# Attention and two gated layers on one Trainium2 core: the setup ahead of the first head, rearranged between VectorE, GpSimd and ScalarE

## The chip, the cores and the metric

The kernel runs on one core of a Trainium2 chip. The metric is the device time of one execution in microseconds (us). A core has TensorE (PE, with its weight loads PEld), VectorE (DVE), ScalarE (ACT), GpSimd (POOL) and SyncE (SP), which here issues the DMAs. The engines run their own instruction lists and wait for one another by semaphores.

## What is computed

Causal attention with a decay bias over 32 heads (4 batches of 8, 576 tokens, head size 64), then two gated layers over 2304 tokens. The part that matters here is the bias, which comes from a running sum over each head's `s`:

```python
scores = scale * np.matmul(q, k.transpose(0, 1, 3, 2))
s_pos = np.maximum(s, 0.0)
cum = np.cumsum(s_pos, axis=-1)
bias = -(cum[:, :, :, None] - cum[:, :, None, :])
scores = np.where(causal, -1000000000.0, scores + np.minimum(bias, 0.0))
scores = scores - np.max(scores, axis=-1, keepdims=True)
attn = np.exp(scores)
attn = attn / (np.sum(attn, axis=-1, keepdims=True) + 1e-09)
x = np.matmul(attn, v)               # then heads side by side: [2304, 512]
h = x @ w_in                         # softmax gate, normalisation, @ w_out
h = maximum(x @ w1, x @ w2, x @ w3)  # second layer, @ w_out2
```

## The kernel before

Every product is made from a high and a low part, so each q, k, v, probability and weight is split in two. One head's attention is spread over three slots of a software pipeline (`slot(t, ...)` on each engine): scores and exponentials of head t, transposes of head t-1, values of head t-2. After the attention come the first layer in six groups of 384 tokens and the second layer in six groups.

The bias is folded into the scores matmul. Four rows beside the 64 rows of q and k in the tile `qk_b` (q_b and k_b are its left and right parts) hold ones, the running sum and its negative, each in high and low parts. For all 32 heads these rows are built once, in the tile `setup` (32 partitions, 8 rows of 576): ones in rows 0, 2, 5, 7 (`one_rows`), `cum_hi` and `cum_lo` in rows 1 and 3, and their negatives `ncum_hi` and `ncum_lo` in rows 4 and 6. The first two heads get their four rows straight from `setup` (L309); the whole tile is then stored to DRAM (L310), and later heads are loaded from there (L299).

Line numbers here are those of the kernel before. Its setup, engine by engine:

- DVE sets the four rows of ones (L1027), waits for `s`, takes its positive part (L1032), makes the running sum with a scan (L1034), splits it (L1036 writes `cum_hi`, L1038 `cum_lo`), then zeroes the 64 columns ahead of `q_a` and `q_b` in both buffers (L1040, L1041). Next is `q_low(0, 0)` (L1047), which waits for POOL's `q_hi_ready`.
- ACT writes `ncum_hi` once `cum_hi` is there (L828) and `ncum_lo` once `cum_lo` is there (L830); each raises `cum_ready`. Its next work is the first exponential (L846).
- POOL zeroes `qk_b` in both buffers (L696, semaphore `rows_zeroed`), zeroes and fills the identities and the mask (L698 to L705), two constants (L707, L708), and then begins on head 0: `qk_high` (L716 q_a, L717 k_a, L718 q_b) and `k_low` (L722), then the same for head 1.
- SP issues `s`, then q/k and v of heads 0 and 1, waits for `rows_zeroed` and for `cum_ready` at 2, and issues the rows of heads 0 and 1 (L309), the store of `setup` (L310) and `g_ln` (L311). `reload(2, ...)` comes after that and waits for POOL's and DVE's splits of head 0.
- PE waits for `setup_pool` at 5 and `setup_dve` at 1. Its first work, `scores_4(0)`, then waits for the high and low parts of q and k of head 0 and for `aux_loaded[0]`, the semaphore of L309.

Of the kernel before, what the change touches and what calls it, by code (L numbers as in the profile page):

```python
# [8 lines left out]
ALU = mybir.AluOpType  # L9
ACT = mybir.ActivationFunctionType  # L10
# [25 lines left out]

def attention_and_mlp(nc, qkT, v, s, w_in, w_out, g_ln, w1, w2, w3, w_out2, out):
    HEADS, D, _, S = qkT.shape
    DM, FF = w_in.shape
    FF2 = w1.shape[1]  # L40
# [4 lines left out]
    PAD = P - S % P  # L45
    NCH = (S + PAD) // P
    SP = S + PAD
# [35 lines left out]
    with ExitStack() as ctx:  # L83
        def sem(name):
            return ctx.enter_context(nc.semaphore(name))
# [7 lines left out]
        def sb(stack, name, shape, dt=F32):  # L93
            return stack.enter_context(nc.sbuf_tensor(name, shape, dt))
# [22 lines left out]
        with ExitStack() as a:  # L117
# [9 lines left out]
            q_a = [sb(a, f"q_a{i}", [P, SP], F32R) for i in range(2)]  # L127
            qk_b = [sb(a, f"qk_b{i}", [P, SP + S], F32R) for i in range(2)]
# [7 lines left out]
        q_b, k_b = [t[:, 0:SP] for t in qk_b], [t[:, SP:SP + S] for t in qk_b]  # L136

        one_rows = [setup[:, i, :] for i in (0, 2, 5, 7)]
        cum_hi, cum_lo, ncum_hi, ncum_lo = [setup[:, i, :] for i in (1, 3, 4, 6)]
# [40 lines left out]
        pool_passed = sem("pool_passed")  # L180
        setup_pool = sem("setup_pool")
        rows_zeroed = sem("rows_zeroed")
        setup_dve = sem("setup_dve")
        cum_step = sem("cum_step")
        cum_ready = sem("cum_ready")
# [85 lines left out]
        f32 = lambda t: t.bitcast(F32)  # L271
# [10 lines left out]
        def _(sp):  # L282
# [20 lines left out]
            load_qk(1, 1)  # L303
            load_v(1, 1)
            sp.wait_ge(rows_zeroed, 2)
            sp.wait_ge(cum_ready, 2)
            for h in range(2):
                rows = setup[h:h + 1, :, :].rearrange("a (r i) s -> a r (i s)", i=2)
                sp.dma_start(f32(qk_b[h][D:D + 4, PAD:SP + S]), rows).then_inc(aux_loaded[h], 16)  # L309
# [382 lines left out]

        @block.gpsimd
        def _(pool):
            for i in range(2):
                pool.memset(f32(qk_b[i][:, PAD:SP + S]), 0.0).then_inc(rows_zeroed, 1)  # L696
            for m in (ident, ident_b, mask):
                pool.memset(m[:, :], 0.0).then_inc(pool_zeroed, 1)  # L698
            pool.wait_ge(pool_zeroed, 3)
# [6 lines left out]
                                   pattern=[[-1, m1 - m0]], channel_multiplier=1).then_inc(setup_pool, 1)  # L706
            pool.memset(one[:, :], 1.0).then_inc(setup_pool, 1)  # L707
            pool.memset(half[:, :], -0.5).then_inc(setup_pool, 1)  # L708

            def qk_high(t, par, known):  # L710

                pool.wait_ge(qk_loaded[par], (t - par) * 16 + 32)
                if known is None or known >= 2:
                    pool.wait_ge(scores_done, 3 * (t - 1))
                pool.sem_inc(pool_passed, 1)
                pool.tensor_scalar(q_a[par][:, PAD:SP], q_raw[par][:, :], SCALE, 1.0, ALU.mult, ALU.mult).then_inc(q_hi_ready, 1)  # L716
                pool.tensor_scalar(k_a[par][:, :], k_raw[par][:, :], 1.0, 1.0, ALU.mult, ALU.mult).then_inc(k_hi_ready, 1)  # L717
                pool.tensor_scalar(q_b[par][0:D, PAD:SP], q_raw[par][0:D, :], SCALE, 1.0, ALU.mult, ALU.mult)  # L718
# [7 lines left out]
                pool.tensor_tensor(v_hl[par][:, :, D:2 * D], v_raw[par][:, :, :], f32(v_hl[par][:, :, 0:D]),  # L726
                                   ALU.subtract).then_inc(v_lo_ready, 1)

            pool.wait_ge(rows_zeroed, 2)
            pool.sem_inc(pool_passed, 1)  # L730
            qk_high(0, 0, 0)
            k_low(0, 0)

# [90 lines left out]

        @block.scalar
        def _(act):
            act.wait_ge(cum_step, 4)
            act.activation(ncum_hi, cum_hi, ACT.Copy, scale=-1.0).then_inc(cum_ready, 1)  # L828
            act.wait_ge(cum_step, 5)
            act.activation(ncum_lo, cum_lo, ACT.Copy, scale=-1.0).then_inc(cum_ready, 1)  # L830

            def split_v(h, par, known):
                act.wait_ge(v_loaded[par], (h - par) * 16 + 32)
                if known is None or known >= 2:
                    act.wait_ge(pv_done, 2 * (h - 1))
                act.activation(v_hl[par][:, :, 0:D], v_raw[par][:, :, :], ACT.Copy).then_inc(v_hi_ready, 1)
# [188 lines left out]
        def _(dve):  # L1025
            for row in one_rows:
                ms = dve.memset(row, 1.0)  # L1027
            ms.then_inc(cum_step, 1)


            dve.wait_ge(s_loaded, 16)
# [4 lines left out]
            dve.tensor_copy(cum_hi.bitcast(F32R), cum).then_inc(cum_step, 1)  # L1036
            dve.wait_ge(cum_step, 4)
            dve.tensor_tensor(cum_lo, cum, cum_hi, ALU.subtract).then_inc(cum_step, 1)  # L1038
            for i in range(2):
                dve.memset(f32(q_a[i][:, 0:PAD]), 0.0)  # L1040
                ms = dve.memset(f32(q_b[i][:, 0:PAD]), 0.0)  # L1041
            ms.then_inc(setup_dve, 1)

            def q_low(t, par):

# [226 lines left out]
```

## Time and profile before

| what | us |
|---|---|
| median of 3 runs | 763.42 |
| lowest and highest run | 762.37, 765.75 |
| the execution that was profiled | 765.75 |
| its span, first to last instruction | 764.0 |
| PE busy | 719.5 (94%) |
| DVE, ACT, POOL busy | 399.0, 321.8, 247.1 |
| mean granted TensorE clock | 0.991 of full speed |

The profiled execution is the slowest of the three; 1.75 us of its 765.75 us lie outside its span. Times in the rows of the trace are counted from the start of the span. An instruction's row gives its start, its duration, engine, line, operation and shapes; in square brackets stands the idle time of the engine ahead of it and what ended it. Successive durations on one engine may overlap a little, so the distance from start to start is what one instruction costs the next.

### The profile page before, as it was taken

Reading aid. Unit: us, or ns where it says so; the run is one execution under the profiler, and the core shown is the slowest. Engines: PE = TensorE matmul, PEld = TensorE weight load, DVE = VectorE, ACT = ScalarE, POOL = GpSimd, SP = SyncE. Lnnn points to the kernel's source line nnn. Section 1 sums busy time; section 2 is a strip of 40 time slices with the busy share of each in tenths; the row PEclk is TensorE's granted clock in tenths of the full one; section 3 lists DMA queues with packets and bytes.
Section 4 is the critical chain, followed back from the end, with each engine's and each line's share of the span. In section 5 each row is a group of like instructions: output and inputs, shape, how many; then the busy total and the mean of one; then the engine's idle time right before and its main releaser. Section 6 shows DMA issues by size and latency. Waiting matters only on the chain.

```text
span 764.0 us, 12615 instructions
## 1 busy us (share of the span) xinstructions
PE 719.5 (94%) x4248; PEld 664.7 (87%) x4248; DVE 399.0 (52%) x700; ACT 321.8 (42%) x765; POOL 247.1 (32%) x248
## 2 busy tenths in 40 slices
PE   3989999998888799999999999999999999999997
PEld 3878888887876698989797999989999999899995
DVE  7979989999865855444535355503213122132120
ACT  3878888888763343332424234312112121121111
POOL 8766679898767432605010100000000000000000
PEclk9999999999999899999999999999999999999999
DMA  8679879889578030720000031000010000100101
GB/s 177 158 165 207 198 182 196 183 198 215 119 176 180 3 83 1 171 79 1 0 0 0 0 111 56 1 27 15 1 42 1 15 27 1 41 0 0 41 0 41
DMA packets 58227, 59.42 MB, mean 78 GB/s; under 512 B 23572, under 2 KB 45204, under 8 KB 58164
## 3 DMA queue, kind: packets, MB, share of 16 engines
q1 hardware_dynamic: 58196, 59.02, 33.1%
q8 instruction: 18, 0.29, 0.2%
q14 instruction: 13, 0.11, 0.1%
HBM read 44.15 MB, written 10.10 MB: 71 GB/s over the span
## 4 chain that ended last, share of the span: by engine, by line
PE 72%; DVE 8%; DMA 5%; issue 4%; ACT 4%; SPq 4%; POOL 2%; DVEq 0%; POOLq 0%; ACTq 0%
PE ps L654 10%; PE ps L653 10%; PE ps L652 10%; PE ps L585 5%; PE ps L587 4%; PE ps L586 4%; PE ps L573 3%; PE ps L574 3%; PE ps L575 3%; PE ps L665 3%; PE ps L666 3%; PE ps L667 3%; DMA qk_b<-aux_dram 3%; PE ps L484 2%; PE ps L598 2%
## 5 line engine op out<-in xcount | busy, mean ns | idle before, releaser
L654 PE MATMUL ps<-x_lo,w_hi 128*128 (+1 forms) x432 | 144.4, 334 | 0.0
L652 PE MATMUL ps<-x_hi,w_hi 128*128 128x384 f32 x432 | 144.4, 334 | 0.0
L653 PE MATMUL ps<-x_hi,w_lo 128*128 128x384 f32 x432 | 144.4, 334 | 0.0
L846 ACT ACTIVATE probs<-ps,nmax 128x576 f32<-128x576 f32 (+4 forms) x160 | 82.8, 537 | 6.8 <-DVE nmax L1054 6.8
L484 PE MATMUL ps<-ident,probs 128*128 128x128 f32 x480 | 77.4, 286 | 8.0 <-DVE pt_lo L1061 4.9
L1061 DVE TENSOR_TENSOR pt_lo<-ps,pt_hi 128x512 fp32r<-128x512 f32 (+1 forms) x128 | 78.3, 652 | 8.6 <-ACT pt_hi L856 5.7
L466 PE MATMUL ps<-k_a,q_a 128*128 128x288 f32 (+2 forms) x192 | 64.0, 341 | 19.3 <-DMA qk_b<-setup 10.9
L652 PEld LDWEIGHTS ps<-x_hi,w_hi 128*128 128x128 f32 x432 | 81.1, 188 | 0.2
L653 PEld LDWEIGHTS ps<-x_hi,w_lo 128*128 128x128 f32 x432 | 81.1, 188 | 0.2
L654 PEld LDWEIGHTS ps<-x_lo,w_hi 128*128 128x128 f32 x432 | 81.1, 188 | 0.0
L1054 DVE TENSOR_REDUCE nmax<-ps 128x1 f32<-128x576 f32 (+4 forms) x160 | 70.5, 483 | 13.1 <-PE ps L471 12.1
L856 ACT ACTIVATE pt_hi<-ps 128x512 fp32r<-128x512 f32 (+1 forms) x128 | 69.7, 573 | 11.7 <-PE ps L484 9.6
L983 ACT ACTIVATE m_hi<-stage 128x384 fp32r<-128x384 f32 x36 | 18.9, 525 | 124.8 <-DVE stage L1217 124.8
L491 PE MATMUL ps<-pt_hi,v_hl 128*128 128x288 f32 (+4 forms) x256 | 68.0, 292 | 0.5 <-issue 0.5
L585 PE MATMUL ps<-lnT_hi,wout_hi 128*128 128x384 f32 x192 | 65.1, 339 | 2.6 <-DVE lnT_lo L1162 2.6
L484 PEld LDWEIGHTS ps<-ident,probs 128*128 128x128 f32 x480 | 52.1, 143 | 16.2 <-DVE pt_lo L1061 10.5
L587 PE MATMUL ps<-lnT_lo,wout_hi 128*128 128x384 f32 x192 | 64.8, 337 | 0.0
L586 PE MATMUL ps<-lnT_hi,wout_lo 128*128 128x384 f32 x192 | 64.8, 337 | 0.0
L1219 DVE TENSOR_TENSOR m_lo<-stage,m_hi 128x384 fp32r<-128x384 f32 x36 | 20.1, 557 | 82.2 <-ACT m_hi L983 82.2
L492 PE MATMUL ps<-pt_lo,v_hl 128*128 128x288 f32 (+4 forms) x256 | 61.7, 288 | 0.0
L573 PE MATMUL ps<-win_hi,x_hi 128*128 128x512 f32 x144 | 56.9, 395 | 4.5 <-DVE ln L1146 2.3
L466 PEld LDWEIGHTS ps<-k_a,q_a 128*128 128x128 f32 x192 | 38.0, 198 | 25.1 <-issue 18.4
(100 smaller groups left out, 1452.3 us busy)
## 6 DMA issues: line engine op xcount, KB each, us to landing
qk_raw<-in_qk_dram SPq DMA_DIRECT2D x64, 288.0 KB, 4.5
xT<-halves SPq DMA_DIRECT2D x32, 144.0 KB, 2.7
xb_dram<-halves SPq DMA_DIRECT2D x32, 144.0 KB, 2.5
xb<-xb_dram SPq DMA_DIRECT2D x24, 192.0 KB, 3.7
rinvB<-rsum_dram SPq DMA_DIRECT2D x24, 192.0 KB, 4.6
stage<-in_moe_w_dram SPq DMA_DIRECT2D x18, 256.0 KB, 4.6
out_dram<-stage SPq DMA_DIRECT2D x18, 256.0 KB, 2.0
v_raw<-in_v_dram SPq DMA_DIRECT2D x32, 128.0 KB, 4.1
```

The source lines that it names most:

```text
L466: pe.matmul(o, q_a[par][:, cols], k_a[par][:, k0:k1], start=start, stop=False)
L484: mm = pe.transpose(ps[:, GBANK[g], P * n:P * (n + 1)], probs[1 - par][:, o:o + P], ident[:, :])
L573: pe.matmul(dst, x_hi[ab][:, c, :], win_hi[:, c, cols], start=(c == 0), stop=False)
L585: pe.matmul(dst, wout_hi[:, f, cols], lnT_hi[:, f, :], start=(f == 0), stop=False)
L586: pe.matmul(dst, wout_lo[:, f, cols], lnT_hi[:, f, :], start=False, stop=False)
L587: mm = pe.matmul(dst, wout_hi[:, f, cols], lnT_lo[:, f, :], start=False, stop=(f == FB - 1))
L652: pe.matmul(dst, w_hi[f][:, i, c, :], x2_hi[par][:, c, :], start=(c == 0), stop=False)
L653: pe.matmul(dst, w_lo[f][:, i, c, :], x2_hi[par][:, c, :], start=False, stop=False)
L654: mm = pe.matmul(dst, w_hi[f][:, i, c, :], x2_lo[:, c, bass.ds(g * GT, GT)], start=False, stop=(c == KC - 1))
L846: act.activation(dst, SCORES[c], ACT.Exp, bias=nmax[par][:, c:c + 1], accum_out=sums_all[:, c, bass.ds(t, 1)]).then_inc(exp_done, 1)
L1054: dve.tensor_reduce(nmax[par][:, c:c + 1], SCORES[c], AX_XY if c == NCH - 1 else AX_X, ALU.max, negate=True).then_inc(max_done, 1)
L1061: dve.tensor_tensor(pt_lo[1 - par][:, o:o + n], ps[:, GBANK[g], 0:n], f32(pt_hi[1 - par][:, o:o + n]), ALU.subtract).then_inc(pt_lo_done, 1)
```

## The change

Four things are edited, all ahead of the first head:

- `ncum_hi` and `ncum_lo` are written by DVE (two multiplications by -1) and no longer by ACT. `cum_ready` is raised once, by the second; SP waits for it at 1.
- DVE's four short memsets of the columns ahead of `q_a` and `q_b` move from behind the splits of the running sum to ahead of its first step.
- POOL's two memsets of `qk_b` move from the front of its program to behind the identities, the mask and the constants.
- POOL's wait for its own memsets, which stood at the head of the work on head 0, now follows them directly.

```diff
             sp.wait_ge(rows_zeroed, 2)
-            sp.wait_ge(cum_ready, 2)
+            sp.wait_ge(cum_ready, 1)
...
         def _(pool):
-            for i in range(2):
-                pool.memset(f32(qk_b[i][:, PAD:SP + S]), 0.0).then_inc(rows_zeroed, 1)
             for m in (ident, ident_b, mask):
...
             pool.memset(half[:, :], -0.5).then_inc(setup_pool, 1)
+            for i in range(2):
+                pool.memset(f32(qk_b[i][:, PAD:SP + S]), 0.0).then_inc(rows_zeroed, 1)
+            pool.wait_ge(rows_zeroed, 2)
+            pool.sem_inc(pool_passed, 1)
...
-            pool.wait_ge(rows_zeroed, 2)
-            pool.sem_inc(pool_passed, 1)
             qk_high(0, 0, 0)
...
         def _(act):
-            act.wait_ge(cum_step, 4)
-            act.activation(ncum_hi, cum_hi, ACT.Copy, scale=-1.0).then_inc(cum_ready, 1)
-            act.wait_ge(cum_step, 5)
-            act.activation(ncum_lo, cum_lo, ACT.Copy, scale=-1.0).then_inc(cum_ready, 1)
...
             ms.then_inc(cum_step, 1)
+            for i in range(2):
+                dve.memset(f32(q_a[i][:, 0:PAD]), 0.0)
+                ms = dve.memset(f32(q_b[i][:, 0:PAD]), 0.0)
+            ms.then_inc(setup_dve, 1)
...
             dve.tensor_tensor(cum_lo, cum, cum_hi, ALU.subtract).then_inc(cum_step, 1)
-            for i in range(2):
-                dve.memset(f32(q_a[i][:, 0:PAD]), 0.0)
-                ms = dve.memset(f32(q_b[i][:, 0:PAD]), 0.0)
-            ms.then_inc(setup_dve, 1)
+            dve.tensor_scalar(ncum_hi, cum_hi, -1.0, None, ALU.mult)
+            dve.wait_ge(cum_step, 5)
+            dve.tensor_scalar(ncum_lo, cum_lo, -1.0, None, ALU.mult).then_inc(cum_ready, 1)
```

DVE at the start of its program, before. `xT` holds `s` and the running sum at this time, `setup` the rows described above, and the two `qk_b` memsets are the columns ahead of q_b:

```order
L1027 MEMSET setup 32x576 x4
L1032 TENSOR_SCALAR xT<-xT 32x576 [waits s_loaded]
L1034 SCALAR_TENSOR_TENSOR xT<-setup,xT 32x576 [waits cum_step]
L1036 CAST setup<-xT 32x576 [waits cum_step]
L1038 TENSOR_TENSOR setup<-xT,setup 32x576 [waits cum_step]
L1040 MEMSET q_a 128x64
L1041 MEMSET qk_b 128x64
L1040 MEMSET q_a 128x64
L1041 MEMSET qk_b 128x64
L1047 SCALAR_TENSOR_TENSOR q_a<-qk_raw,q_a 64x576 [waits q_hi_ready]
```

The same stretch of DVE in the changed kernel:

```order
L1022 MEMSET setup 32x576 x4
L1025 MEMSET q_a 128x64
L1026 MEMSET qk_b 128x64
L1025 MEMSET q_a 128x64
L1026 MEMSET qk_b 128x64
L1031 TENSOR_SCALAR xT<-xT 32x576 [waits s_loaded]
L1033 SCALAR_TENSOR_TENSOR xT<-setup,xT 32x576 [waits cum_step]
L1035 CAST setup<-xT 32x576 [waits cum_step]
L1037 TENSOR_TENSOR setup<-xT,setup 32x576 [waits cum_step]
L1038 TENSOR_SCALAR setup<-setup 32x576
L1040 TENSOR_SCALAR setup<-setup 32x576 [waits cum_step]
L1045 SCALAR_TENSOR_TENSOR q_a<-qk_raw,q_a 64x576 [waits q_hi_ready]
```

The four short memsets went up past the running sum, and two instructions of 32x576 stand between the split of the sum and `q_low(0, 0)`.

POOL at the start of its program, before, from its first work to the first instruction on head 0:

```order
L696 MEMSET qk_b 128x1152 x2
L698 MEMSET ident 128x128
L698 MEMSET ident_b 128x128
L698 MEMSET mask 128x320
L701 ISA [waits pool_zeroed]
L701 AFFINE_SELECT ident<-ident 128x128
L701 AFFINE_SELECT ident_b<-ident_b 128x128
L705 AFFINE_SELECT mask<-mask 128x128 x2
L705 AFFINE_SELECT mask<-mask 128x64
L707 MEMSET one 128x1
L708 MEMSET half 128x1
L716 TENSOR_SCALAR q_a<-qk_raw 128x576 [waits rows_zeroed,qk_loaded0]
```

The end of that stretch on POOL in the changed kernel:

```order
L699 AFFINE_SELECT ident<-ident 128x128
L699 AFFINE_SELECT ident_b<-ident_b 128x128
L703 AFFINE_SELECT mask<-mask 128x128 x2
L703 AFFINE_SELECT mask<-mask 128x64
L705 MEMSET one 128x1
L706 MEMSET half 128x1
L708 MEMSET qk_b 128x1152 x2
L718 TENSOR_SCALAR q_a<-qk_raw 128x576 [waits rows_zeroed,qk_loaded0]
```

The two long memsets now stand last, right ahead of the work on head 0. The instruction lists of SP and PE are the same as before.

## Rows read from the trace of the kernel before

**Rows 1.** The page's part on the chain that ended last
```profile
PE 72%; DVE 8%; DMA 5%; issue 4%; ACT 4%; SPq 4%; POOL 2%; DVEq 0%; POOLq 0%; ACTq 0%
```
**Rows 2.** The chain in order of time, 0 to 30 us: start, us, what
```profile
3.71 1.41 DVE xT L1034
...
6.41 0.69 ACT setup L830
7.18 3.63 DMA qk_b<-setup
...
10.95 0.58 PE ps L466
...
14.92 0.77 DVE nmax L1054 x2
```
**Rows 3.** Timeline of DVE, 0 to 7.5 us
```profile
3.20 0.48 DVE L1032 TENSOR_SCALAR xT<-xT 32x576 f32<-32x576 f32 x1
5.15 0.45 DVE L1036 CAST setup<-xT 32x576 fp32r<-32x576 f32 x1
5.63 0.75 DVE L1038 TENSOR_TENSOR setup<-xT,setup 32x576 f32<-32x576 f32 x1
6.34 0.11 DVE L1040 MEMSET q_a<- 128x64 f32 x1
6.41 0.11 DVE L1041 MEMSET qk_b<- 128x64 f32 x1
7.48 1.21 DVE L1047 SCALAR_TENSOR_TENSOR q_a<-qk_raw,q_a 64x576 fp32r<-64x576 f32 x1 [0.81 <-POOL q_a L716]
```
**Rows 4.** Timeline of SP's issues, 0 to 40 us
```profile
5.52 0.59 SPq L295 DMA_DIRECT2D v_raw<-in_v_dram  x1
7.18 1.44 SPq L309 DMA_DIRECT2D qk_b<-setup  x2
```
**Rows 5.** DMA, issue to landing: load of s, L290 (0 to 3 us), L295 (4 to 6 us)
```profile
xT<-in_s_dram SPq DMA_DIRECT2D x1, 72.0 KB, 1.9
...
L290 SPq DMA_DIRECT2D qk_raw<-in_qk_dram x2: 561/576/591, 1.2 to 1.8; - x2
...
DMA to landing us min/median/max: 3.9/4.3/4.8
...
DMA to landing us min/median/max: 5.0/5.0/5.0
```
**Rows 6.** Timeline of POOL, 0 to 11 us
```profile
0.73 2.05 POOL L696 MEMSET qk_b<- 128x1152 f32 x2 [0.29 <-POOLq L1261]
...
3.62 0.29 POOL L701 TENSOR_SCALAR_AFFINE_SELECT ident<-ident 128x128 f32<-128x128 f32 x1 [0.25 <-POOL mask L698]
3.87 1.34 POOL L701 TENSOR_SCALAR_AFFINE_SELECT ident_b<-ident_b 128x128 bf16<-128x128 bf16 x1
5.16 1.56 POOL L705 TENSOR_SCALAR_AFFINE_SELECT mask<-mask 128x128 bf16<-128x128 bf16 x3
6.77 0.67 POOL L716 TENSOR_SCALAR q_a<-qk_raw 128x576 fp32r<-128x576 f32 x1
7.42 0.66 POOL L717 TENSOR_SCALAR k_a<-qk_raw 128x576 fp32r<-128x576 f32 x1
8.05 1.16 POOL L718 TENSOR_SCALAR qk_b<-qk_raw 64x576 fp32r<-64x576 f32 x1
9.19 1.39 POOL L722 TENSOR_TENSOR qk_b<-qk_raw,k_a 64x576 fp32r<-64x576 f32 x1
```
**Rows 7.** Line L718 on POOL over 0 to 240 us: shortest, median, longest in ns
```profile
L718 POOL TENSOR_SCALAR qk_b<-qk_raw x32: 661/667/1176, 8.1 to 206.3; 64x576 fp32r<-64x576 f32 x32
```
**Rows 8.** Timeline of ACT, 0 to 14 us: its first work
```profile
0.73 1.28 ACT L828 ACT_TABLE_LOAD   x1 [0.73 <-PEq L1261]
5.63 0.68 ACT L828 ACTIVATE setup<-setup 32x576 f32<-32x576 f32 x1 [3.62 <-DVE setup L1036]
```
**Rows 9.** Waits of PE, 29 to 210 us: us in total, times, longest
```profile
PE ps L466 <- DMA qk_b<-aux_dram: 6.6, 6, 2.9
```

## The prediction, made before the changed kernel was run

> **What bounds the kernel now.** I read the chain that ended last first, by engine: 72% of it is PE, and no other engine has more than 8% [rows 1]. So the change can act only through the time at which PE gets its first work, and through what a later or earlier start does to the pipeline behind it. The same chain in order of time shows how the first 11 us go: DVE makes the running sum (scan from 3.71), ACT writes the last negated row from 6.41 for 0.69, SP issues the rows of head 0 at 7.18, that transfer takes 3.63, and PE starts at 10.95 [rows 2]. From 14.92 on the chain is DVE, ACT and PE work of heads 0 and 1, each item waiting for the one before, so a shift of PE's first matmul is handed on whole.
>
> Two other things end close to that transfer. POOL's last step on head 0, `k_low`, starts at 9.19 and takes 1.39, so it ends at 10.58 [rows 6]. PE waits for it too. The transfer ends at 7.18 + 3.63 = 10.81 [rows 2], so `k_low` has a slack of only 0.23. DVE's `q_low(0, 0)` ends at 7.48 + 1.21 = 8.69 [rows 3], 2.1 ahead of the transfer. So PE starts at the later of transfer and `k_low`, plus 0.14 (10.81 to 10.95).
>
> **When the negated rows are ready.** Removed from ACT: two activations, of which only the second (0.69) lies on the chain. Added on DVE: two one-input instructions of 32x576. DVE has two rows of that size and kind, 0.48 and 0.45; the two-input form took 0.75 [rows 3]. I take 0.45 each, since the cast is nearest (it also reads one row of `setup` and writes another), with 0.75 as the upper bound and 0.3 as the lower (what is left if the fixed part of each overlaps its neighbour). Moved on DVE: four short memsets, which start 0.07 apart (6.34, 6.41) [rows 3], 4 x 0.07 = 0.28, now ahead of the sum; they delay it by all of that, because DVE went from the ones straight into L1032 at 3.20 without an idle time [rows 3].
>
> So `cum_lo`, which DVE left for the next instruction at 6.34, is now left at 6.62, and with 2 x 0.45 `ncum_lo` is done at about 7.55, if nothing disturbs DVE. Before it was done at 6.41 + 0.69 = 7.10. The edit that is meant to skip an engine makes the rows ready 0.45 later, not earlier.
>
> **What a later issue costs.** SP would issue at 7.63 instead of 7.18. Bounds: all of it, 0.45, if the transfer takes 3.63 again; nothing, if the transfer was waiting behind others. For the second speaks that the load of `s`, 72 KB, four times the 4 x 1152 words of four bytes of this transfer, and first in the queue, landed 1.9 after its issue, and that the last piece of v of head 1, issued at 5.52, took 5.0, so that it landed at 10.52, 0.3 ahead of our transfer [rows 4, 5]. The small transfer stood behind the loads of head 1. Issued at 7.63 with 1.9 for itself it would land at 9.5, well before these loads are through. I take 0 here: the landing stays at about 10.8, until the issue is later than 10.8 - 1.9 = 8.9.
>
> **POOL's order.** The memsets of `qk_b` take 2.05 together [rows 6]. With them last, the identities and the mask start at 0.73 and, undisturbed, take about 0.25 each (3.62 to 3.87 for the first [rows 6]); all of that is done near 3.0, and the memsets near 5.1. Before, POOL came to head 0 at 6.77. It can't gain the 1.7 us: the second copy of head 0's q and k was issued at 1.8 and landed 4.8 later, at 6.6 [rows 5]. The gain is at most 0.1 to 0.2. The wait that now stands behind the memsets has nothing late behind it: what is queued there is `q_a` of head 0, which the load holds until 6.6 anyway. SP's wait for `rows_zeroed` ends at 5.1 instead of 2.8, ahead of the 7.6 at which SP is let go by `cum_ready`. PE's waits on `setup_pool` and `setup_dve` both end sooner. ACT's table load ran at 0.73, 4.9 ahead of the activation it belongs to [rows 8]; it stays first in ACT's list, without a wait, so I cost it at nothing.
>
> **What DVE and POOL do to each other.** This is the term that I take as deciding. Three rows show POOL standing still beside a DVE instruction. The select of `ident_b` took 1.34 where its wider-typed twin took 0.29, and it ended 0.1 behind DVE's scan (3.71 + 1.41) [rows 2, 6]. The three mask selects took 1.56 together beside DVE's cast and subtract. The 64x576 multiply L718 took 1.16 beside `q_low(0, 0)` (7.48 to 8.69), where its median is 0.667 [rows 3, 6, 7]. And `q_low` itself took 1.21 where a two-input instruction of that width took 0.75, with `k_a` on POOL until 8.05 [rows 3, 6]. The two take turns.
>
> Before, DVE was idle for 0.81 ahead of `q_low` while POOL did `q_a` [rows 3]. Now the two multiplications lie just there. In turns, from the time at which `cum_lo` is done: `ncum_hi` 6.62 to 7.07 (POOL, ready at 6.77, waits 0.30); `q_a` 0.65 to 7.72; `ncum_lo` 0.45 to 8.17; `k_a` 0.63 to 8.80; `q_low` 0.64 to 9.44; `qk_b` 0.50 to 9.94; `k_low` 1.39 to 11.33. POOL's steps are the distances between its starts, `q_low` is what was left of it after `k_a` (8.05 to 8.69), `qk_b` what was left after `q_low` (8.69 to 9.19) [rows 3, 6]. `k_low` ends at 11.33, 0.75 later than before, and is now the last of PE's waits. `cum_ready` comes at 8.17, SP issues at 8.25, still short of 8.9, and the transfer lands at 10.8. PE starts at 11.33 + 0.14 = 11.47, **0.5 later** than 10.95. If the two multiplications don't hold POOL up, `k_low` ends at 10.6 and PE starts at 10.95: 0. Between these ends I take 0.5, since the cast, the row most like them, stood beside a held-up select.
>
> `k_low` of head 1 and SP's reload of head 2 each follow 0.75 later. The next scores begin when PE is through with head 0's, so they are shifted by the same 0.5 to 0.75.
>
> **Sum.** 765.75 for the profiled execution + 0.5 = 766.25. That execution is the slowest of three; against the median, 763.42 + 0.5 = **763.9**.
>
> **The rivals.**
>
> 1. *All hidden.* The transfer lands as before and the multiplications don't hold POOL: 763.4. For it: two of the four terms are covered by the loads of head 1. Against it: the held-up selects.
>
> 2. *The long memsets hold DVE too.* They now run from about 3.0 to 5.1, and DVE's L1032 is due at 3.48. Were that instruction to wait for the first memset to end at 4.0, the sum would be 0.5 later, the subtract would run to 7.15, and the turns would be `q_a` to 7.8, `ncum_hi` to 8.25, `k_a` to 8.9, `ncum_lo` to 9.35, `qk_b` to 9.85 or 10.0, `q_low` to 10.6, `k_low` to 12.0: PE starts 1.2 later. SP issues at 9.4, past 8.9, and the transfer lands between 11.3 (at 1.9) and 13.0 (at 3.63), the latter 2.1 later than before. The case gives 764.6 to 765.5. The trace can't decide it: POOL's long memsets ran there beside DVE memsets only. The Trainium skill (SBUF — State Buffer, Who interferes with whom) says that a VectorE instruction in a two-port mode, a one-input multiply among them, and any GpSimd instruction block each other whole, while a two-input VectorE instruction blocks only GpSimd instructions that read; by that rule this rival is what happens.
>
> 3. *Slower by more than can be missed.* PE stood 6 times for the bias rows of later heads, up to 2.9 at once, 6.6 in all [rows 9]. These rows stand in SP's queue behind the reloads, and SP is let go by POOL's splits. If the later POOL start pushes such a load behind a large one in two more slots, that is 2 x 2.9 = 5.8 more: 769.7. It decides from two new stalls on. Against it: POOL's lag is under 1 us, and the largest stall needs a weight load of the same moment.
>
> 4. *Faster by the same mechanism.* The 2.9 stall goes: 763.9 - 2.9 = 761.0; and all six together would give 757.3.
>
> **How the numbers follow.** Forecast (0.3 to 0.8 later) 0.42; rival 1 0.2; rival 2 0.3; rival 3 0.03; rival 4 0.05, of it 0.01 with more than the one stall. A difference of 0.5% (3.8 us) is about what a measurement of this kernel can tell from no change. Forecast, rivals 1 and 2 and most of rival 4 lie within it: 0.96. Faster 0.01, slower 0.03. The range: the likely cases span 763.4 to 765.5; the three runs before lie 1.1 below and 2.3 above their median, and I allow 1.9 below the lowest case and 1.0 above the highest, which also takes in a part of rival 4: 761.5 to 766.5.
>
> **What would show it.** PE's first matmul at about 11.5, with POOL's `k_low` of head 0 ending at 11.3 and the transfer from `setup` landing earlier. The issue of that transfer between 7.6 and 8.3. POOL's selects at 0.25 each, `q_a` of head 0 near 7.1. If DVE's L1031 in the changed kernel lasts about 1.0 in place of 0.48, rival 2 is right. If the transfer takes under 3 us from its issue, the reading of the queue is right; if it takes 3.6 again, that reading is wrong and PE's start moves with the issue. A stall of PE on the bias rows that comes or goes after 30 us would be larger than all of this.

## The result, and the profile after

| | before | after |
|---|---|---|
| median of 6 runs, us | 763.09 | 768.61 |
| lowest and highest | 762.37, 765.75 | 764.22, 770.58 |
| ratio, 95% interval | | 1.0065 (1.0037 to 1.0093) |
| profiled execution, its span | 765.75, 764.0 | 766.72, 764.9 |

The changed kernel is 0.65% slower, about 5 us (the two medians are 5.5 apart). The forecast was 763.9, no measurable difference. The two profiled executions differ by only 0.9 us in span; why so little is the first thing that the experiments had to settle.

The timeline of the changed kernel from 2.8 to 15 us, DVE, POOL and SP together (start, duration, engine, line, operation, idle time ahead). It answers to [rows 3, 4, 6]:

```profile
2.86 2.05 POOL L708 MEMSET qk_b<- 128x1152 f32 x2
3.50 1.72 DVE L1031 TENSOR_SCALAR xT<-xT 32x576 f32<-32x576 f32 x1
...
6.55 0.67 POOL L718 TENSOR_SCALAR q_a<-qk_raw 128x576 fp32r<-128x576 f32 x1 [1.64 <-DMA qk_raw<-in_qk_dram]
6.63 0.90 DVE L1035 CAST setup<-xT 32x576 fp32r<-32x576 f32 x1
7.20 0.86 POOL L719 TENSOR_SCALAR k_a<-qk_raw 128x576 fp32r<-128x576 f32 x1
7.57 1.09 DVE L1037 TENSOR_TENSOR setup<-xT,setup 32x576 f32<-32x576 f32 x1
8.03 1.16 POOL L720 TENSOR_SCALAR qk_b<-qk_raw 64x576 fp32r<-64x576 f32 x1
8.59 0.91 DVE L1038 TENSOR_SCALAR setup<-setup 32x576 f32<-32x576 f32 x1
9.16 1.59 POOL L724 TENSOR_TENSOR qk_b<-qk_raw,k_a 64x576 fp32r<-64x576 f32 x1
9.43 2.27 DVE L1040 TENSOR_SCALAR setup<-setup 32x576 f32<-32x576 f32 x1
10.73 0.66 POOL L718 TENSOR_SCALAR q_a<-qk_raw 128x576 fp32r<-128x576 f32 x1
...
11.79 1.44 SPq L309 DMA_DIRECT2D qk_b<-setup  x2
...
13.27 0.44 SPq L310 DMA_DIRECT2D aux_dram<-setup  x1
...
14.28 2.73 SPq L290 DMA_DIRECT2D qk_raw<-in_qk_dram  x2
14.28 0.58 PE L466 MATMUL ps<-k_a,q_a 128*128 128x288 f32 x1 [14.28 <-DVE rinvT L1078]
```

DVE's first step on the sum lasted 1.72 instead of 0.48: it was issued at 3.50 and ended at 5.22, behind both long memsets of POOL (2.86 to 4.9). The cast then took 0.90 beside POOL's `q_a`. The second multiplication took 2.27: it stood through `k_low` of head 0 and `q_a` of head 1 and ended at 11.70. So the negated rows were ready 4.6 us later than before (7.10), and SP issued them at 11.79 instead of 7.18. PE began at 14.28 instead of 10.95. The profile puts PE's wait down to a DVE memset that ended at the same moment. PE doesn't wait for that memset at this place. It waits for the transfer from `setup`, issued 2.49 us earlier, the same distance as in e1 and e3 below, where the profile names the transfer.

SP's list matters more. Behind its wait for `cum_ready` stand the store of all heads' rows and the load of head 2's q and k. That load went out at 14.28 instead of 10.66. The chain of waits of the changed kernel, 13 to 26 us, runs through it and not through PE's first matmul:

```profile
14.28 2.09 SPq L290
...
16.41 4.74 DMA qk_raw<-in_qk_dram
...
21.36 0.68 POOL q_a L718
22.04 0.02 issue
22.07 1.21 DVE q_a L1045
...
23.30 1.42 DVE nmax L1052 x3
...
24.76 0.70 DVE pt_lo L1059
...
25.50 1.77 PE ps L484 x7
```

POOL began on head 2 at 21.36, five us later than in the kernel before. PE ran out of work meanwhile. Stretches of 17 to 23 and 23 to 29 us (length; busy time and count of PE, PEld, DVE, ACT, POOL; granted clock, DMA share, GB/s), the changed kernel:

```profile
17.00:23.00 6.00, 4.32 (x29) 3.87 (x27) 2.44 (x5) 3.96 (x13) 1.64 (x3) 1.00 0.83 200
23.00:29.00 6.00, 2.85 (x12) 2.52 (x12) 5.33 (x11) 3.74 (x12) 6.00 (x7) 0.72 0.41 99
```

The second of them in the kernel before (its second profile, of which more below), and from PE's timeline of the changed kernel the wait in it:

```profile
23.00:29.00 6.00, 4.75 (x37) 4.33 (x38) 5.78 (x11) 4.94 (x16) 4.62 (x7) 1.00 0.81 169
```

```profile
25.50 1.75 PE L484 MATMUL ps<-ident,probs 128*128 128x128 f32 x7 [2.95 <-DVE pt_lo L1059]
```

PE did 12 matmuls where it had done 37, and the granted clock stood at 0.72 of full speed in that stretch, a mixture of its two levels of 1.2 and 2.4 GHz. Ahead of the row at 25.50 PE had been idle for 2.95 us.

### The profile page after: what moved, and what is told of

It is laid out like the page before. It is cut to its first block, busy times and chain, and to the rows that moved or that the text cites. A ratio compares the mean times of both kernels' runs of the same rounds, so it can differ in the third digit from the quotient of the medians.

```text
span 764.9 us, 12615 instructions
## 1 busy us (share of the span) xinstructions
PE 718.6 (94%) x4248; PEld 663.6 (87%) x4248; DVE 403.4 (53%) x702; ACT 320.7 (42%) x763; POOL 245.9 (32%) x248
## 4 chain that ended last, share of the span: by engine, by line
PE 73%; DVE 10%; SPq 5%; DMA 4%; issue 4%; ACT 3%; POOL 1%; DVEq 0%; ACTq 0%; POOLq 0%
PE ps L652 10%; PE ps L654 10%; PE ps L653 10%; PE ps L585 5%; PE ps L587 4%; PE ps L586 4%; PE ps L573 4%; PE ps L575 4%; PE ps L574 4%; PE ps L665 3%; PE ps L666 3%; PE ps L667 3%; DMA qk_b<-aux_dram 2%; PE ps L484 2%; DVE nmax L1052 2%
```

## The experiments

Two numbers are given for each kernel's profile: when POOL starts on head 2 (its `q_a`), and the **lag**: how much later than in the second profile of the kernel before ACT starts the first exponential (576 columns wide) of a head. Ratios are to the kernel before, run in the same rounds; the quotients of the medians differ from them by up to 0.001. Each profile is of one execution. Those of e1 and e8 were the fastest of their kernel (764.82 and 762.57), so their later lags may be short of the usual.

| kernel | PE starts | head 2 on POOL | lag, head 4 | lag, head 27 | ratio (95%) |
|---|---|---|---|---|---|
| before, again | 10.89 | 16.48 | 0 | 0 | 1.0003 (0.9986 to 1.0019) |
| after | 14.28 | 21.36 | +4.83 | +4.48 | 1.0065 (1.0037 to 1.0093) |
| e1, POOL's part | 11.95 | 18.58 | +2.10 | +5.28 | 1.0067 (1.0047 to 1.0088) |
| e2, DVE's part | 11.32 | 16.66 | +0.16 | +0.82 | 1.0029 (1.0008 to 1.0049) |
| e3, rows late | 13.68 | 20.34 | +5.27 | +6.20 | 1.0067 (1.0042 to 1.0091) |
| e4, PE late | 13.02 | 17.14 | +0.65 | -0.03 | 1.0004 (0.9988 to 1.0020) |
| e8, loads late | 10.86 | 19.01 | +2.51 | +3.19 | 1.0058 (1.0032 to 1.0084) |
| e6, e1 with two-input step | 10.74 | 16.59 | +0.10 | -0.20 | 0.9995 (0.9976 to 1.0014) |
| e7, after with two-input step | 11.14 | 17.79 | +2.63 | +3.16 | 1.0041 (1.0018 to 1.0063) |
| g1, store behind | 10.85 | 15.84 | -0.64 | -0.94 | 0.9998 (0.9978 to 1.0019) |
| g2, after, store behind | 14.16 | 18.40 | +1.90 | +1.85 | 1.0042 (1.0022 to 1.0063) |
| f1, rows ahead of v | 11.14 | 16.49 | -0.02 | -0.89 | 0.9960 (0.9942 to 0.9979) |
| g3, g1 and f1 | 10.88 | 15.95 | -1.32 | -3.04 | 0.9965 (0.9950 to 0.9980) |
| f2, after and f1 | 14.15 | 20.97 | +5.84 | +3.59 | 1.0038 (1.0018 to 1.0058) |
| f4, e1 and f1 | 11.52 | 18.07 | +1.57 | -0.77 | 1.0005 (0.9987 to 1.0024) |

**What the first profile of the kernel before hid.** The same kernel, profiled again:

> The kernel before, unchanged, profiled a second time: it tells what the first profile of it hid. Theory A (the late start is kept to the end): the first profile was of the slowest execution, with one 2.9 us stall of PE on the bias rows near 43 us that the usual execution does not have; then this profile has a span near 761 to 762 us, no stall over 1.5 us on these rows before 50 us, and the exponential of head 20 near 140.5 instead of 143.2. Theory B (the late start is made good in the loop over heads, since its loads set the pace there, and the 5 us of the median come from something later, the clock for one): head 20 stands at 143.2 again whatever happens before it. Timed against itself the ratio is 1.000 within 0.3%.

Its span was 760.1 instead of 764.0. The timeline of PE in the first profile has this row:

```profile
42.91 0.40 PE L466 MATMUL ps<-k_a,q_a 128*128 128x288 f32 x1 [2.89 <-DMA qk_b<-aux_dram]
```

The second profile has no wait for these rows above 1.0. The exponential of head 5 starts at 48.68 in the first, at 44.63 in the second (ACT's timeline of each):

```profile
48.68 0.73 ACT L846 ACTIVATE probs<-ps,nmax 128x576 f32<-128x576 f32 x1
```

```profile
44.63 0.74 ACT L846 ACTIVATE probs<-ps,nmax 128x576 f32<-128x576 f32 x1
```

The 4.05 us between them are still 4.05 at head 27. The first profile was of the slowest execution, and this stall with what followed it (the granted clock was 0.76 from 41 to 47 us) hid the lag: against the second profile the changed kernel is 4.8 us longer, which agrees with the ratio. This is what theory A expected; the comparison of the first two profiles (lag 4.96 at head 4, 0.1 at head 17) would have led to theory B.

**The two halves of the change.** e1 moves only POOL's memsets; e2 makes only the edits on DVE, ACT and SP.

```diff
 e1:
-            for i in range(2):
-                pool.memset(f32(qk_b[i][:, PAD:SP + S]), 0.0).then_inc(rows_zeroed, 1)
             for m in (ident, ident_b, mask):
...
             pool.memset(half[:, :], -0.5).then_inc(setup_pool, 1)
+            for i in range(2):
+                pool.memset(f32(qk_b[i][:, PAD:SP + S]), 0.0).then_inc(rows_zeroed, 1)
+            pool.wait_ge(rows_zeroed, 2)
+            pool.sem_inc(pool_passed, 1)
...
-            pool.wait_ge(rows_zeroed, 2)
-            pool.sem_inc(pool_passed, 1)
             qk_high(0, 0, 0)
```

> Only POOL's two memsets of qk_b moved to the end of its setup; the negated rows stay on ACT and DVE is as before. DVE's first step of the running sum (L1032, 0.48 before) waits for both memsets, from 3.2 to about 4.9, and lasts about 1.9; cum_lo is done near 8.4 instead of 6.3, cum_ready near 9.2 instead of 7.1, PE starts at 11.3 to 11.8 instead of 10.95, and the load of head 2, issued at 10.66 before, goes out near 11.8. Theory A: median 1 to 1.5 us above before. Theory B: no difference. If the memsets do not hold DVE, L1032 lasts 0.5 and PE starts at 10.95.

> Only the negated rows moved from ACT to DVE, and DVE's four short memsets moved ahead; POOL is as before, its long memsets first. L1032's counterpart lasts 0.5 again. The two multiplications by -1 must take turns with POOL's work on head 0. If turns alternate, cum_ready comes at 8.2, the transfer lands at about 10.8 and PE starts at 11.5; if the last one is held until k_low of head 0 and q_a of head 1 are through, as in the profile of the changed kernel, cum_ready comes at about 11.5 and PE starts at 14. Theory A: median above before by what head 2 is late, 0.7 or 4 to 5 us. Theory B: no difference.

In e1 the step on DVE stood still again, as its timeline shows:

```profile
2.86 2.06 POOL L708 MEMSET qk_b<- 128x1152 f32 x2
3.20 2.02 DVE L1032 TENSOR_SCALAR xT<-xT 32x576 f32<-32x576 f32 x1
```

SP issued the rows at 9.46 and PE began at 11.95. The shift at the start was as expected, the median was not: 4.8 us above before instead of 1 to 1.5. In its profile the lag was 2.1 at head 4, 3.2 at head 5 and 5.7 at head 9. The largest step, ahead of head 9, was a stall of PE on the bias rows, with the clock at half level behind it (PE's timeline, then the stretches 65 to 69, 69 to 73 and 73 to 77 us):

```profile
69.38 0.44 PE L466 MATMUL ps<-k_a,q_a 128*128 128x288 f32 x1 [1.52 <-DMA qk_b<-aux_dram]
```

```profile
65.00:69.00 4.00, 2.78 (x22) 2.23 (x20) 3.85 (x9) 3.83 (x12) 1.65 (x3) 1.00 1.10 203
69.00:73.00 4.00, 3.62 (x17) 3.48 (x18) 1.88 (x3) 0.60 (x4) 3.06 (x3) 0.57 0.72 135
73.00:77.00 4.00, 4.00 (x32) 3.61 (x32) 2.71 (x6) 3.88 (x10) 2.42 (x4) 1.00 0.44 100
```

Whether the other executions of e1 had such a stall isn't known. In e2 POOL came to head 0 at 7.14, when the second multiplication was nearly through, so only `q_a` met it (0.80 instead of 0.67):

```profile
6.45 0.53 DVE L1038 TENSOR_SCALAR setup<-setup 32x576 f32<-32x576 f32 x1
6.91 0.48 DVE L1040 TENSOR_SCALAR setup<-setup 32x576 f32<-32x576 f32 x1
7.14 0.80 POOL L716 TENSOR_SCALAR q_a<-qk_raw 128x576 fp32r<-128x576 f32 x1
7.48 1.44 SPq L309 DMA_DIRECT2D qk_b<-setup  x2
...
11.32 0.58 PE L466 MATMUL ps<-k_a,q_a 128*128 128x288 f32 x1 [11.32 <-POOL qk_b L722]
```

Neither of the expected orders came about. PE started 0.4 later than before, released by `k_low`: what the forecast had described for the whole change. The 2.27 of the second multiplication needs both halves: DVE late by the memsets, and the multiplications on DVE. The ratio of e2 is above 1 by 0.08 to 0.49% although head 2 came to POOL only 0.2 late; no run explains it.

**Is it the late rows alone?** e3 leaves DVE and POOL as they were and delays only `cum_ready`.

```diff
             act.wait_ge(cum_step, 5)
+            for _i in range(7):
+                act.activation(<unused columns of xT>, cum_hi, ACT.Copy, scale=-1.0)
             act.activation(ncum_lo, cum_lo, ACT.Copy, scale=-1.0).then_inc(cum_ready, 1)
```

> The kernel before, with seven more activations on ACT ahead of ncum_lo that write into unused columns (7 x 0.68 = 4.8 us), so that cum_ready comes at 11.8, as in the changed kernel, while DVE and POOL do just what they did before. PE starts near 14.2, SP issues the load of head 2 near 14.3 instead of 10.66, and head 2 is about 5 us late. Theory A: median 4 to 5.5 us above before, as the changed kernel. Theory B: no difference, or under 1 us. A third, that the loss comes from DVE and POOL holding each other up rather than from the late rows: no difference either.

SP issued the rows at 11.19, and the lag at head 4 (+5.3) and the ratio (1.0067) are close to those of the changed kernel (+4.8, 1.0065). That DVE and POOL hold each other up costs, as far as these times can tell, only through the semaphore that SP waits for.

**PE's start or SP's loads?** e4 delays PE alone; e8 lets the rows of heads 0 and 1 go on time and holds SP behind them.

```diff
 e4:
+            for _i in range(10):
+                act.activation(<unused columns of xT>, ...).then_inc(late, 1)
...
+            pe.wait_ge(late, 10)
             scores_4(0, 0, 0)
 e8:
+            for _i in range(7):
+                act.activation(<unused columns of xT>, ...).then_inc(late, 1)
...
+            sp.wait_ge(late, 7)
             sp.dma_start(aux_dram, setup[:, :, :]).then_inc(aux_stored, 16)
```

> The kernel before, with ten more activations on ACT behind ncum_lo that write into unused columns, and PE waits for the last of them ahead of its first matmul. The rows of the bias, SP's issues, POOL and DVE's setup are as before; only PE starts late, near 13.3 (the activations start 0.58 apart). SP's load of head 2 goes out at 10.66. Theory A1, what counts is that the loads of head 2 go out late: head 2 is then late only by what PE itself is late, 2.5, and the median is at most 2.5 us above before. Theory A2, any late start of the first head is kept and grows in the loop over heads, since PE meets the loads of the bias rows at another moment: 4 us or more above before.

> The kernel before, with seven more activations on ACT behind ncum_lo, and SP waits for the last of them (about 11.2) between the rows of heads 0 and 1 and the store of the rows of all heads. PE starts at 10.95 as before; the store and the load of head 2 go out 2.5 to 3 us later. Theory A1: head 2 is late by nearly 3, and the median is about 3 us or more above before. Theory A2 (only the first matmul counts): no difference.

The two come out opposite. With PE's first matmul 2.1 us late and the loads on time, the lag was 2.0 at head 0, 0.7 at head 2 and gone by head 27, and the ratio was 1.0004: at most 0.2% (1.5 us) above before. With PE on time and the loads late, POOL waited for head 2 in the timeline of e8:

```profile
11.13 0.37 SPq L312 DMA_DIRECT2D aux_dram<-setup  x1
...
12.08 4.00 SPq L291 DMA_DIRECT2D qk_raw<-in_qk_dram  x4
...
19.01 0.67 POOL L718 TENSOR_SCALAR q_a<-qk_raw 128x576 fp32r<-128x576 f32 x1 [4.61 <-DMA qk_raw<-in_qk_dram]
```

and the time was 0.58% above before. The load went out only 1.4 us later than before, but POOL had it 2.5 us later. The distance between store and load goes with it: from the issue of the load to POOL's start took 5.8 us with the store 2.0 ahead of it (before), 6.6 to 7.1 with the store 0.95 to 1.0 ahead (e1, e3, e7, e8, f2, f4 and the changed kernel), and 5.2 with the store behind it (g1, g2 below).

PE shows the difference too. Stretches of 17 to 23 and 23 to 29 us of e4, then of e8:

```profile
17.00:23.00 6.00, 4.21 (x32) 3.62 (x32) 5.41 (x10) 4.88 (x16) 5.86 (x7) 1.00 0.32 75
23.00:29.00 6.00, 4.63 (x37) 4.08 (x36) 5.76 (x11) 4.98 (x16) 4.59 (x7) 1.00 0.79 181
```

```profile
17.00:23.00 6.00, 2.13 (x18) 1.90 (x16) 3.22 (x5) 2.81 (x7) 3.99 (x5) 1.00 0.53 117
23.00:29.00 6.00, 5.15 (x31) 4.77 (x32) 5.36 (x10) 3.97 (x14) 4.51 (x6) 0.72 0.65 133
```

In e4 PE's longest wait there was 1.3 us and the granted clock stayed at 1.00. In e8 PE stood 4.0 us before 23.15 and then ran in part at the lower level. So the assumption under the whole prediction, that the change acts through PE's first matmul, doesn't hold. e8 holds back the store, `g_ln` and the load of head 2 together; g2 below puts the load of head 2 ahead of the other two.

**Do the long memsets hold every DVE instruction?** e6 is e1, e7 the changed kernel, both with a two-input form of the first step and the same result:

```diff
-            dve.tensor_scalar(s_sb, s_sb, 0.0, None, ALU.max).then_inc(cum_step, 1)
+            dve.wait_ge(cum_step, 1)
+            dve.scalar_tensor_tensor(out=s_sb, in0=s_sb, scalar=0.0, in1=one_rows[0],
+                                     op0=ALU.max, op1=ALU.mult).then_inc(cum_step, 1)
```

> As the kernel in which only POOL's memsets were moved, but DVE takes the positive part of s with a two-input instruction (max with 0, then times the row of ones), result unchanged. If a long memset on POOL holds only DVE's one-input instructions, this step lasts 0.75 instead of 2.02 and starts at 3.2, cum_ready comes at 7.3 instead of 9.4, POOL reaches head 0 at 6.6 as before, PE starts near 10.9 and the median is within 0.7 us of before. If memsets hold any DVE instruction, the step lasts about 2 again and the median is 4 to 5 us above before.

> The changed kernel with the same two-input form for the positive part, and nothing else. The step lasts 0.75 instead of 1.72, cum_lo is done near 7.0 instead of 8.66. The two multiplications then meet POOL's q_a and k_a of head 0. If they alternate, cum_ready comes at 8.2 to 8.5, PE starts at 11.5 and the median is 1 to 2 us above before; if the second is again held until k_low is through, cum_ready comes at 11 or later, PE starts near 13.5, and the median is 4 to 5 us above before.

The timeline of e6, beside the same memsets:

```profile
2.86 2.05 POOL L708 MEMSET qk_b<- 128x1152 f32 x2
...
3.39 0.75 DVE L1033 SCALAR_TENSOR_TENSOR xT<-xT,setup 32x576 f32<-32x576 f32 x1
...
4.17 1.34 DVE L1035 TENSOR_TENSOR_SCAN xT<-setup,xT 32x576 f32<-32x576 f32 x1
```

The two-input step and the scan ran beside the memsets undisturbed, and the whole cost of e1 was gone (0.9995). The rule that rival 2 quoted from the Trainium skill (SBUF — State Buffer, Who interferes with whom) agrees with both traces: a one-input VectorE instruction in a two-port mode and a GpSimd one block each other whole, while a two-input one clashes only with GpSimd instructions that read, which a memset doesn't. The page speaks of a wait for one instruction; here the step waited for two memsets in a row (2.02 in e1). In e7 the two multiplications did alternate with POOL (0.92 and 0.91), `cum_ready` came at 8.5, the load of head 2 went out at 11.08; the store stood right ahead of it, and 1.3 us on POOL and 3.4 us in the median remained. In its profile the lag was 2.7 at head 2, more than POOL's 1.3: PE stood 2.54 us before 21.93, and the granted clock was 0.51 from 23 to 29 us.

**The store in SP's list.** g1 and g2 put the store and `g_ln` behind head 2's load, in the kernel before and in the changed one.

```diff
-            sp.dma_start(aux_dram, setup[:, :, :]).then_inc(aux_stored, 16)
-            sp.dma_start(g_sb[:, :], g_ln).then_inc(g_loaded, 16)
...
             reload(2, 0, 2)
+            sp.dma_start(aux_dram, setup[:, :, :]).then_inc(aux_stored, 16)
+            sp.dma_start(g_sb[:, :], g_ln).then_inc(g_loaded, 16)
             reload(3, 1, 3)
```

> The kernel before with one move in SP's list: the store of the rows of all heads (576 KB) and g_ln are issued behind the load of head 2's q and k instead of ahead of it. That load goes out at 10.66 as before, with nothing large ahead of it, and lands in 3 to 4 us instead of 5.8. Theory A1 (the time at which POOL can begin on head 2 sets the pace for the loop): q_a of head 2 starts at 15 to 15.5 instead of 16.5, and the median is 0.5 to 1.5 us below before. If nothing is to be had below 16.5, since the scores of head 0 then hold POOL, no difference. A cost is possible: the bias rows of head 2 wait for the store, which lands 2 us later; if PE meets that, 1 to 2 us above.

> The changed kernel with the same move in SP's list. cum_ready is as late as before the move, 11.7, and PE starts at 14.2, but the load of head 2 goes out at 13.3 instead of 14.3, ahead of the store. Theory A1: q_a of head 2 starts near 17.5 to 18 instead of 21.4, and the median comes down from 5 us to 2 to 4 us above before. Theory A2 (the late first matmul, or DVE and POOL holding each other up, costs the time): the median stays 5 us above before.

In g2 PE still began at 14.16, but POOL had head 2 at 18.40 instead of 21.36. The lag fell from 4.8 to 1.9, with the granted clock at 1.00 all through 17 to 35 us. The time fell from 5 to 3.2 us above before, but the two intervals overlap (1.0037 to 1.0093 and 1.0022 to 1.0063), so that this step is shown by the lag and not by the time. In the kernel before the move brought head 2 forward by 0.6 and the median not at all.

**The rows of later heads ahead of v.** f1 is the kernel before with this edit in `reload`, f2 the changed kernel with it, f4 is e1 with it, g3 is f1 and g1.

```diff
-                if known is None or known >= 4:
-                    reload_v(t - 2, par)
                 if known == 3:
                     sp.wait_ge(aux_stored, 16)
                 if known is None or known >= 3:
                     reload_aux(t - 1, 1 - par)
+                if known is None or known >= 4:
+                    reload_v(t - 2, par)
```

> The kernel before, with the load of the bias rows of head t-1 issued ahead of the load of v of head t-2 in every turn of SP's loop. PE waits 3.2 to 6.6 us in all on these rows while the heads run; the rows would land about 1 us sooner. If these waits add to the time, the median is 1 to 4 us below before; if they are slack that the next wait takes up, no difference; if v then comes late for ACT, 1 us above.

> Both moves in SP's list on the kernel before. The candidate for a version that beats both: the sum of the two, 0 to 4 us below before.

> The changed kernel with the bias rows of head t-1 loaded ahead of v of head t-2, as in the kernel that came out 0.4% below before. Theory K (kept): what the late load of head 2 costs, 5 us at head 2, stays in full until the end, and only the waits of the loop go: the ratio to before is 1.0065 - 0.004 = 1.0025. Theory G (grown): part of the 5 us is made in the loop, where PE, being late, meets the rows of the bias behind the loads of v; with the rows first, head 3 is still 5 us late but the ratio falls to 1.000 or below.

> Only POOL's memsets moved, and the bias rows loaded ahead of v. Without the second edit head 2 was 1.7 us late and head 9 already 5.7 us, the median 4.8 above before. Theory K: 1.7 to 5 us above the kernel with the second edit alone (759.6): 761.3 to 764.6, and the lag at head 9 is still 3 or more above that at head 2. Theory G: the lag stays near 2 us from head 2 to head 31, and the median is 760.5 to 761.7.

f1 is faster than both kernels: 759.63 against 762.72, 0.40% (0.21 to 0.58) less than before, clear of zero but under the half per cent that the prediction named as its bound. g3 is no better. In f1's profile PE waited for the rows only twice (2.6 the longer), 3.0 us in all; the second profile of the kernel before has six such waits and 3.2. Where the gain sits can't be read from one profile of each.

f2 is 1.0038 and f1 0.9960, so the edits of the change cost 0.78%, 6 us (4 to 8 by the two intervals), on top of f1 too: all that it was late at head 4 (5.8). By the medians theory G, which had 1.000 or below, is out. f4 against f1 is 0.45%, 3.4 us, where its lag over f1 at head 4 was 1.6: theory G had 0.9 to 2.1 us and theory K 1.7 to 5. The two intervals together leave 1.4 to 5.4 us, so the time doesn't decide between them. The profile of f4 bears out neither: the lag didn't grow between heads 2 and 9 (1.69, 1.52), as it had in e1 (1.67, 5.66), which speaks against K, and it was gone at head 27 (-0.77, f1 -0.89), which speaks against G. Single profiles of the kernel before differ by up to 4 us from head 5 on.

## Why the prediction was wrong, point by point

- *"So the change can act only through the time at which PE gets its first work"* is the step that failed, and with it *"a shift of PE's first matmul is handed on whole"*. e4 moved that time by 2.1 us at no cost that shows, and only 0.7 of it was left at head 2; e8 left it alone and cost 0.58%. The path that costs is POOL's start on head 2, and that hangs on SP. The prediction put SP's reload of head 2 at 0.75 late, behind POOL's split, and gave no price to the load's own place behind SP's wait. From the issue of the rows to that load SP needs 2.49 us (11.79 to 14.28), so with the predicted issue at 8.25 the load could have gone out at 10.74, no later than before: the path came to matter only because the rows were 3.5 us later than predicted, the next point. In the runs, kernels with head 2 on POOL by 17.1 (e4, e6) cost nothing, e2 with 16.66 cost 0.29% (0.08 to 0.49), and those at 17.8 or later 0.4 to 0.7%, leaving aside f2 and f4, which carry the gain of f1. The cost isn't in proportion to the delay: e1, 2.1 late on POOL, lost as much as the changed kernel, 4.9 late.
- *DVE and POOL take turns*: the mechanism was right, the size was not, and this is the second step that failed: `cum_ready` at 8.17 by the turns, 11.70 measured. With PE 3.3 us later (14.28 and 10.95) the prediction's own sum gives 763.4 + 3.3 = 766.7, just outside its range. `cum_lo` came at 8.66 instead of 6.62, since the first step waited for both memsets (1.72 for the 0.48 of [rows 3]) and the cast for `q_a`. Rival 2 had named this and let it wait for the first memset only. Turns were not strict either: DVE got its turn between `q_a` and `k_a`, `k_a` and `qk_b`, `qk_b` and `k_low`, but not between the two memsets nor between `k_low` and the next `q_a`, which POOL did back to back. That last miss is worth 0.65 of the 2.27.
- *The multiplications take 0.45 each*: 0.53 and 0.48 where nothing disturbed them (e2), 0.91 and 2.27 in the changed kernel.
- *The transfer waited behind the loads of head 1*: right. Issued 4.6 us later, it let PE begin 2.5 after its issue, where before PE began 3.8 after it.
- *POOL can't gain from its order; ACT's table load stays hidden*: right. `q_a` of head 0 began at 6.55 instead of 6.77, the selects took 0.25 to 0.29, and the table load ran at 0.73.
- *The range*: worked out from cases that all ended with PE's first matmul. Rival 3, slower by stalls on the bias rows, came near the size (5.8) by luck: PE's waits for bias rows took 3.1 us in the changed kernel's profile, against 3.2 in the second profile of the kernel before. It had been given 3%.
- *The sum against one profiled execution*: the profile held a 2.9 us stall that the usual execution doesn't have. The prediction counted the 6.6 us of such waits as the kernel's own; the second profile has 3.2.

**What stays open.** Why the loss doesn't follow the delay. e1 loses 4.8 us in the median with a lag of 2.1 at head 4 (its profile had 5.3 at head 27, 2.8 of it from the stall shown above); f4 against f1 has 3.4 with 1.6. PE's clock takes a part in it. In the changed kernel, e3, e7, e8, f2 and f4 PE stood 2.5 to 4.0 us ahead of the first transposes that wait for DVE, at 21 to 26 us, and the granted clock then fell, to between 0.51 and 0.81 in the stretch 23 to 29 us; in e1, e2, e4, g1 and g2 the same wait was 0.5 to 1.4 and the clock stayed at 1.00. A wait alone doesn't decide it: the clock fell after one of 1.52 in e1, and not after one of 1.53 in the kernel before. The mean granted clock over all timed executions is 0.988 in e1 and f4, where the kernel before has 0.991, f1 0.992 and e4 0.992; the others with a late head 2 have 0.987 to 0.991 too. As an estimate from these figures, PE at the lower clock for 2 x 0.003 of 764 us loses half of 4.6, 2.3 us, which would be the right size for e1. But the clock falls in the changed kernel's profile where PE has stood still, before head 4, so it is already within that lag, and the sum for the changed kernel would come out too large. How much of each loss is the delay and how much the clock that falls with it was not separated. Nor was it tested why DVE gets no turn between two memsets.

## What to carry to other kernels

When an edit makes a semaphore later, list everything that stands behind the wait in the queue of the engine that waits, and follow each item to its own user: here the first matmul, which waits for the late transfer, could start 2 us late at no cost that shows, while holding back what only stood behind that transfer cost 0.58%. Ask of a late start whether it delays the first item of a pipeline (which later items can take up) or a buffer's reload that later items need. Profile the kernel before more than once when a change is worth less than its spread: one stall of 2.9 us in the base profile, with what followed, hid nearly all of a loss of 5.

## What the runs showed of the hardware

- A GpSimd memset of 128x1152 (1.0 us each) held a one-input 32x576 step of DVE from 3.20 to 5.22, two memsets long, and let a two-input step (0.75) and a scan (1.34) pass.
- With DVE and POOL both ready they took turns after most instructions, but twice in the changed kernel POOL did two in a row while DVE stood: the two memsets (a step of 0.48 lasted 1.72), and `k_low` with the next `q_a` (a multiplication of 0.48 lasted 2.27).
- The landing of a load of two copies of 288 KB went with the place of a 576 KB store from SBUF to DRAM: from the issue of the load to the engine's start 5.8 us with the store 2.0 ahead, 6.6 to 7.1 with 0.95 to 1.0 (seven profiles), 5.2 with the store behind the load.
- After PE had stood 2.95 us in the changed kernel, the granted clock was 0.72 over 23 to 29 us; after 2.54 in e7 it was 0.51; in e4, whose longest wait there was 1.27, it stayed at 1.00.
